# Token-mixing kernel: the phase angles of groups 3 to 21 as three one-pass products of split operands instead of one product in plain float32

## The reference

```python
# 1: causal 7-tap mix over tokens, one softmaxed set of taps per head
out = np.einsum('hk,bskhg->bshg', w, x_unf)
# 2: a phase per element, then two token-by-token mixes (4224 x 4224)
theta = x @ w_theta                       # 192 x 192
cos_t, sin_t = (np.cos(theta), np.sin(theta))
zr = x * cos_t
zi = x * sin_t
yr = np.einsum('ts,bsd->btd', w_tok_r, zr)
yi = np.einsum('ts,bsd->btd', w_tok_i, zi)
u = x + yr + yi
x = u + np.maximum(u @ w_ch, 0.0)
# 3: low-rank token mix and a channel MLP
h = xt @ U @ V
u = x + h.transpose(0, 2, 1)
out = u + np.maximum(u @ w_ch1, 0.0) @ w_ch2
```

## Time and profile before

| | |
|---|---|
| median of 3 runs | 2742.34 us (2740.83 to 2742.51) |
| profiled execution, device time | 2744.99 us |
| its span in the trace | 2743.2 us |
| TensorE busy | 2720.2 us, 99% |
| VectorE busy | 2136.2 us, 78% |
| ScalarE busy | 1034.1 us, 38% |
| GpSimd busy | 195.3 us, 7% |

### The profile page before, as it was taken

The page is one execution under the profiler, slowest core; times in us unless marked ns, Lnnn a source line. Parts: engine busy times, 40 slices in busy tenths (PEclk is TensorE's granted clock), DMA queues, the critical chain, the costliest instruction groups (busy, mean ns, idle before and its releaser), DMA issues.

```text
span 2743.2 us, 35814 instructions
## 1 busy us (share of the span) xinstructions
PE 2720.2 (99%) x14519; PEld 2545.2 (93%) x14519; DVE 2136.2 (78%) x2451; ACT 1034.1 (38%) x1392; POOL 195.3 (7%) x228
## 2 busy tenths in 40 slices
PE   8999999999999999999999999999999999999999
PEld 7898999999999999999999999999999889999999
DVE  6888878888798788788887887986767876666665
ACT  6543333333333333333333334333322443344343
POOL 0101101001011011010010010110110000000000
PEclk9999999999999999999999999999999999999999
DMA  5878769678677687697686786775873000000000
GB/s 191 204 186 205 179 194 213 160 198 199 176 202 177 179 203 179 184 220 160 193 203 164 202 193 175 199 189 174 217 153 91 35 3 29 31 29 31 29 31 35
DMA packets 102372, 412.62 MB, mean 150 GB/s; under 512 B 10657, under 2 KB 28737, under 8 KB 102081
## 3 DMA queue, kind: packets, MB, share of 16 engines
q0 software_dynamic: 31680, 151.40, 31.3%
q1 hardware_dynamic: 70528, 258.94, 27.0%
HBM read 371.37 MB, written 38.93 MB: 150 GB/s over the span
## 4 chain that ended last, share of the span: by engine, by line
PE 96%; DVE 2%; issue 1%; ACT 0%; DMA 0%; SPq 0%; DVEq 0%; ACTq 0%
PE bank L1276 24%; PE bank L1277 23%; PE bank L1278 23%; PE bank L1387 2%; PE bank L1391 2%; PE bank L1390 2%; PE bank L1388 2%; PE bank L1389 2%; PE bank L1220 2%; PE bank L1372 2%; PE bank L1375 2%; PE bank L1376 1%; PE bank L1373 1%; PE bank L1374 1%; PE bank L1226 1%; PE bank L1221 1%
## 5 line engine op out<-in xcount | busy, mean ns | idle before, releaser
L1276 PE MATMUL bank<-w_h,z_op 128*128 128x448 f32 (+1 forms) x3465 | 1234.2, 356 | 8.0 <-DVE z_op L931 2.7
L1278 PE MATMUL bank<-w_h,z_op 128*128 128x448 f32 (+1 forms) x3465 | 1227.9, 354 | 0.0
L1277 PE MATMUL bank<-w_l,z_op 128*128 128x448 f32 (+1 forms) x3465 | 1227.7, 354 | 0.0
L586 ACT ACTIVATE w_h<-w_raw 128x1344 fp32r<-128x1344 f32 (+1 forms) x385 | 485.7, 1262 | 1066.8 <-PE bank L1278 939.8
L1276 PEld LDWEIGHTS bank<-w_h,z_op 128*128 128x128 f32 x3465 | 651.8, 188 | 51.2 <-DVE z_op L931 3.0
L1278 PEld LDWEIGHTS bank<-w_h,z_op 128*128 128x128 f32 x3465 | 651.7, 188 | 41.6
L1277 PEld LDWEIGHTS bank<-w_l,z_op 128*128 128x128 f32 x3465 | 651.9, 188 | 40.8
L943 DVE TENSOR_TENSOR w_l<-w_raw,w_h 128x1344 fp32r<-128x1344 f32 (+1 forms) x385 | 567.7, 1475 | 63.4 <-ACT w_h L586 62.6
L561 POOL DMA_DIRECT2D w_raw<-in_w_tok x220 | 192.8, 897 | 1869.6 <-DVE w_l L943 1130.0
L1153 DVE SCALAR_TENSOR_TENSOR hid_l<-bank,hid_h 128x384 fp32r<-128x384 f32 x264 | 144.5, 557 | 152.7 <-ACT hid_h L811 149.5
L979 DVE TENSOR_TENSOR Y<-Y,bank 128x1344 f32<-128x1344 f32 (+1 forms) x105 | 154.8, 1474 | 103.0 <-PE bank L1278 102.2
(11 more groups left out here) (144 smaller groups left out, 2923.4 us busy)
## 6 DMA issues: line engine op xcount, KB each, us to landing
w_raw<-in_w_tok SPq DMA_DIRECT2D x220, 672.0 KB, 4.4
w_raw<-in_w_tok POOLq DMA_DIRECT2D x220, 672.0 KB, 6.7
z_raw<-z_out SPq DMA_DIRECT2D x85, 576.0 KB, 6.7
z_out<-zf SPq DMA_DIRECT2D x65, 384.0 KB, 6.5
x_win<-in_xin SPq DMA_DIRECT2D x22, 585.0 KB, 6.3
out<-res SPq DMA_DIRECT2D x22, 576.0 KB, 2.8
v_raw<-in_v SPq DMA_DIRECT2D x11, 144.0 KB, 3.1
w_raw<-in_w SPq DMA_DIRECT2D x1, 1536.0 KB, 6.4
```

Of the source, the lines that this page charges most:

```text
L586: nc.scalar.activation(w_h[:, s % WRING, :, 0:n], w_raw[:, SLOT[s], :, 0:n], ACT.Copy).then_inc(wh_ready, 1)
L1276: mm(to, zh, wh, start=(k == 0 and not goes_on), stop=False, skip_group_check=goes_on)
L1277: mm(to, zh, wl, start=False, stop=False, skip_group_check=goes_on)
L1278: last = mm(to, zl, wh, start=False, stop=(k == KC - 1), skip_group_check=goes_on)
```

## The change

From group 3 on (`SPLIT_FROM`), a unit's angles are made from split operands. `theta_w` is split once: `theta_h` by ScalarE at stage 19, `theta_l` by VectorE at stage 20. For each unit ScalarE copies the 128 tokens of `attn` into `attn_h`, and VectorE subtracts that from `attn` into `attn_l`, both in the stage before the unit's own and last in their engine's part of it, ScalarE's copy after its `w_hi`. TensorE then runs nine products instead of three. `attn_l` lies where `turns` lies and `attn_h` where `angle` lies, `theta_l` where `theta_w` lies; so the copy waits until the unit before has done with its angles (`angle_step`). Groups 0 to 2 are as before.

```diff
+THETA_SPLIT = 19
+SPLIT_FROM = 3
...
-        theta_w = sb(prep, "theta_w", [P, 4 * D])
+        with ExitStack() as first:
+            theta_w = sb(first, "theta_w", [P, 4 * D])
+        theta_l = sb(prep, "theta_l", [P, 4 * D], F32R)
+        theta_h = sb(prep, "theta_h", [P, 4 * D], F32R)
...
-        turns = sb(prep, "turns", [P, GW])
-        angle = sb(prep, "angle", [P, GW])
+        with ExitStack() as first:
+            turns = sb(first, "turns", [P, GW])
+            angle = sb(first, "angle", [P, GW])
+        attn_l = sb(prep, "attn_l", [P, TP, P], F32R)
+        attn_h = sb(prep, "attn_h", [P, TP, P], F32R)
...
+            def attn_hi_of(m):
+                act.wait_ge(conv_tap, conv_done(m // KC))
+                act.wait_ge(theta_ready, m)
+                act.wait_ge(angle_step, 3 * m)
+                nc.scalar.activation(attn_h[:], attn_of(m), ACT.Copy).then_inc(attn_hi, 1)
...
+                for n in range(SPLIT_FROM, GP):
+                    for r in range(KC):
+                        if theta_stage(n, r) - 1 == s:
+                            attn_hi_of(KC * n + r)
...
+            def attn_lo_of(m):
+                dve.wait_ge(attn_hi, m - KC * SPLIT_FROM + 1)
+                vec.tensor_tensor(attn_l[:], attn_of(m), attn_h[:].bitcast(F32), ALU.subtract).then_inc(attn_lo, 1)
...
+                if s == THETA_SPLIT + 1:
+                    dve.wait_ge(theta_w_hi, 1)
+                    vec.tensor_tensor(theta_l[:], theta_w[:], theta_h[:].bitcast(F32), ALU.subtract).then_inc(theta_w_lo, 1)
...
-                mm(angle_bank, src[:, 1, rows], theta_w[:, D:3 * D], start=True, stop=False)
-                mm(angle_bank[:, 0:D], src[:, 0, rows], theta_w[:, 0:D], start=False, stop=False)
...
-                mm(angle_bank[:, D:GW], src[:, 2, rows], theta_w[:, 3 * D:4 * D], start=False, stop=True)
+                if split_unit(m):
+                    pe.wait_ge(theta_w_lo, 1)
+                    pe.wait_ge(attn_lo, m - KC * SPLIT_FROM + 1)
+                    for t, to, cols in ((1, angle_bank, slice(D, 3 * D)), (0, angle_bank[:, 0:D], slice(0, D)),
+                                        (2, angle_bank[:, D:GW], slice(3 * D, 4 * D))):
+                        ah, al, wh, wl = attn_h[:, t], attn_l[:, t], theta_h[:, cols], theta_l[:, cols]
+                        mm(to, ah, wh, start=(t == 1), stop=False)
+                        mm(to, ah, wl, start=False, stop=False)
+                        mm(to, al, wh, start=False, stop=(t == 2))
```

More of the change, by code:

```diff
@@ L367, in build @@
         theta_ready = sem("theta_ready")
+        theta_w_hi = sem("theta_w_hi")
+        theta_w_lo = sem("theta_w_lo")
+        attn_hi = sem("attn_hi")
+        attn_lo = sem("attn_lo")
         turn_step = sem("turn_step")
@@ L436, in sines_of, with split_unit, attn_of @@
             return sines_1 if m == 1 else sines
+        def split_unit(m):
+            return m >= KC * SPLIT_FROM
+        def attn_of(m):
+            return attn[:, :, (m % KC) * P:(m % KC + 1) * P]
         def theta_bank(m):
@@ L704, in _ @@
                             sin(KC * n + r)
+                if s == THETA_SPLIT:
+                    act.wait_ge(theta_ready, KC * SPLIT_FROM)
+                    nc.scalar.activation(theta_h[:], theta_w[:], ACT.Copy).then_inc(theta_w_hi, 1)
+                for n in range(SPLIT_FROM, GP):
+                    for r in range(KC):
+                        if theta_stage(n, r) - 1 == s:
+                            attn_hi_of(KC * n + r)
                 if s == PER * (CHUNKS - 1) + 4:
@@ L1047, in _ @@
                             products(KC * n + r)
+                if s == THETA_SPLIT + 1:
+                    dve.wait_ge(theta_w_hi, 1)
+                    vec.tensor_tensor(theta_l[:], theta_w[:], theta_h[:].bitcast(F32), ALU.subtract).then_inc(theta_w_lo, 1)
+                for n in range(SPLIT_FROM, GP):
+                    for r in range(KC):
+                        if theta_stage(n, r) - 1 == s:
+                            attn_lo_of(KC * n + r)
                 if s >= 1 and STAGES[s - 1][:2] == (CHUNKS - 1, 5):
@@ L1219, in theta @@
                     pe.wait_ge(product, 2 * m)
-                mm(angle_bank, src[:, 1, rows], theta_w[:, D:3 * D], start=True, stop=False)
-                mm(angle_bank[:, 0:D], src[:, 0, rows], theta_w[:, 0:D], start=False, stop=False)
-                if n == 0:
-                    pe.wait_ge(attn_ready, 1)
-                mm(angle_bank[:, D:GW], src[:, 2, rows], theta_w[:, 3 * D:4 * D], start=False, stop=True)
+                if split_unit(m):
[7 more added lines that the diff above has]
+                        mm(to, al, wh, start=False, stop=(t == 2))
+                else:
+                    mm(angle_bank, src[:, 1, rows], theta_w[:, D:3 * D], start=True, stop=False)
+                    mm(angle_bank[:, 0:D], src[:, 0, rows], theta_w[:, 0:D], start=False, stop=False)
+                    if n == 0:
+                        pe.wait_ge(attn_ready, 1)
+                    mm(angle_bank[:, D:GW], src[:, 2, rows], theta_w[:, 3 * D:4 * D], start=False, stop=True)
                 for t in range(TP):
```

## The result

The changed kernel takes 2800.45 us (median of 4 runs, 2799.43 to 2802.35) against 2741.59 us for the kernel before: a ratio of 1.0215, 95% interval 1.0203 to 1.0226, or +58.9 us. The forecast was +48 us in the terms of the runs (2790, range 2766 to 2829): right in direction and mechanism, 10 us short.

What follows compares the result with a forecast made beforehand. TensorE was taken to bound the kernel. From 2745.0 us: products -6.3, waits +38.9, restarts +3.3, clock +10.2, weight split +0.9 make 2792.0, stated as 2790 us in the runs' terms, range 2766 to 2829.

Steps and rivals of the forecast that it cites:

- Bound: Whole kernel: the time is the sum of TensorE's instructions, and any wait of TensorE adds one for one.
- Products: 57 units from group 3 on: nine one-pass products take 1.18 us instead of 1.29, -6.3 us in all.
- The unit of 1.02 us: Alternative unit time by the Trainium skill's issue gap, 82.5 ns at 192 columns; the products would then give -15 us.
- Waits: TensorE's units waiting for VectorE's subtraction: 38.9 us in 30 waits.
- The pattern of the late groups: Tile 0 of groups 12 to 21: waits of 2.5 us in even and 1.9 in odd groups, 21.9 us.
- the small waits at tiles 1 and 2: Tiles 1 and 2, where VectorE has mostly caught up: eleven small waits, 2.9 us.
- Restarts: After each wait TensorE's next product starts 0.1 us later than usual: 30 x 0.11 = 3.3 us.
- Clock: TensorE's granted clock falls to 1.2 GHz after half of 14 long waits: 7 x 1.45 = 10.2 us.
- Rival 1: The 192-column products aren't taken in one pass, 0.325 us each: +67.6 instead of -6.3, 2863 us; chance 0.12.
- Rival 2: VectorE's lag at tile 0 is made good after TensorE's first wait: 2737 down to 2730 us; chance 0.05.
- No queue cost elsewhere: The per-unit splits cost nothing as busy time on ScalarE or VectorE; no queue of SP or POOL is passed.
- the one-off split of the weights: 768 elements on each engine at stages 19 and 20, while group 3's convolution builds its lag: +0.9 us.

Runs made afterwards that it cites:

- experiment 3: Changed kernel with TensorE still waiting for VectorE's subtraction, but running the three plain products on unsplit theta_w: 2798.67 us, ratio 1.0212.
- experiment 2: Changed kernel with the per-unit splits made, but TensorE neither waiting for nor using them and running the plain products: 2741.38 us, ratio 1.0001.
- experiment 8: Changed kernel with both per-unit splits as early as the buffers allow: 2738.82 us, ratio 0.9993.
- experiments 5 and 4: Changed kernel with filler products ahead of TensorE's long waits, followed by the three plain products (2788.28 us) or by the nine (2781.43 us).
- experiment 6: Changed kernel run once more without an edit, for a second profile: 2796.36 us in one run.
- experiment 4: Changed kernel with 11 or 14 filler products ahead of TensorE's wait at tile 0 of 15 groups: 2781.43 us, ratio 1.0147.
- experiments 1 and 7: Changed kernel with VectorE's subtraction moved ahead of the residual sums (2744.34 us), or with the residual sums one stage later (2745.32 us).

## Why the prediction was right, and where its sizes were off

**Bound.** TensorE's wait came one for one into the time, as put: experiment 3 has the loss with nothing else of the change, experiment 2 has the rest and none of the loss.

**Products.** Forecast -6.3 us, measured -6.6 in the trace (experiment 8's units without a wait: 0.116 us shorter from the last product before the unit to the third behind its first transpose) and -6.85 between experiments 5 and 4. The 0.109 us for a 192-column product was measured as 0.111. That it is the weight load that holds it is likely, but not shown; only that it isn't the columns (0.090 by the line) and hardly hangs on the order. The unit of 1.02 us that the prediction sets beside its own takes the trace's 0.1752 us for the long products and 82.5 ns for the short ones (82.5 ns and its rule for the long ones too would make 0.98); the trace has 111 ns for the short ones, so neither came.

**Waits.** Forecast 38.9 us in 30 units, measured 42.6 in 24. The pattern of the late groups is as worked out, 2.62 and 2.01 us for 2.5 and 1.9, and 3.49 for 3.4 in group 3. Four sizes were off. TensorE's first product starts 0.15 us after the subtraction's end (1201.51 + 0.56 = 1202.07, then 1202.21), not 0.05 as behind L937: 0.1 us in each of 24 waits, 2.3 us. Group 4 waited 2.24 us instead of 0.5. Before, the clock had fallen after the wait that ended at 246.82, and TensorE needed 7.15 us from there to the unit at 253.97; in this profile the same wait left the clock up and it needed 5.6, so it came 1.6 us earlier to the same work of VectorE. Group 7 waited 3.01 us instead of 2.2: ScalarE's `w_h` was late by a transfer of `w_raw`, VectorE stood idle for it two stages ahead of the unit, and what it lost there it brought to the subtraction. Its and ScalarE's rows:

```profile
525.13 1.56 DVE L984 TENSOR_TENSOR w_l<-w_raw,w_h 128x1344 fp32r<-128x1344 f32 x1 [0.76 <-ACT w_h L610]
...
523.77 1.33 ACT L610 ACTIVATE w_h<-w_raw 128x1344 fp32r<-128x1344 f32 x1 [4.47 <-DMA w_raw<-in_w_tok]
```

And the small waits at tiles 1 and 2 came to 2.0 us instead of 2.9: one in group 3 and five of the seven at tile 2 of the even groups from 8 on did not come, since VectorE was just in time (six of the seven came in the second profile, experiment 6).

**Restarts.** Forecast 3.3 us, measured 1.8: 0.076 each, and fewer.

**Clock.** This is the term that was mis-sized: "I take half: 7 x 1.45 = 10.2 us". It was 12 x 1.57 = 18.8 us in the profile, and 19.0 by experiment 4 over all runs. The number of falls was the low factor: long waits were followed by one in four of five cases and not in half. The price was low by little, 1.45 us in place of 1.57, since the count stopped at 251.02, one product short of the end of the period. With 18.8 in place of 10.2 the forecast would have been 2799. The other misses are smaller and partly made each other good: the waits 3.7 us above the forecast, restarts and products 1.5 and 0.3 below it.

**Rival 1** (narrow products in two passes, 2863 us) is excluded by the rows of the unit. **Rival 2** (the lag made good) too: late in the kernel the waits still alternate between 2.62 and 2.01 us, to group 21. It was right that lag is made anew in each group, and experiments 1 and 7 show by what.

**No queue cost elsewhere.** Experiment 2's ratio of 1.0001 covers the load on both engines together; the one-off split of the weights wasn't tried by itself.

## What to carry to other kernels

When a change makes the bounding engine wait for an engine that is 84% busy, that share says little: read at each place how late the other engine ends what stands ahead in its queue, add the new operation, and sum over the places. The same subtraction cost 59 us behind the residual sums and 3 us ahead of them. Count beside each such wait the clock that TensorE loses by standing idle; here it was a third of the loss, and it makes two variants with equal waits differ by several us in either direction. So before a difference of 2 or 3 us is put down to an edit, compare the start-to-start times of products that the edit did not touch.

## What the hardware showed that I had not expected

- TensorE idle for 1.8 us or more in a stream that is otherwise dense was followed by a period of 3.4 us at 1.2 GHz in most cases and not in others of the same length, and the same kernel had 13 or 10 of them in two executions. One costs 1.57 us. Filler in the gap kept the clock at 2.4 GHz.
- At full clock the same dense stream of 448-column products runs at 0.2027 or 0.2067 us a product over some hundred products at a time, up to 4 us in all between two orders of nine products elsewhere.
- A fall of the clock can save a wait later on: 1.6 us at group 4 in the kernel before, as much as the fall cost; where it didn't come, that wait did.
- A one-pass product of 192 columns costs 0.111 us in a row of its like and about 0.11 on the mean in any of the three orders; behind a long one it takes 0.088, and the next long one pays the 0.023 back.
- From VectorE's end to TensorE's first product it took 0.15 us here and 0.05 us behind L937. Dropping the second wait ahead of it, on `theta_w_lo` (experiment 3), did not shorten it; the cause is open.
